# Attention, dense layers and routed experts in one kernel: ScalarE copies the gate columns, and the second batch's first head pair is prepared in the dense stage

## What is computed

```python
for t in range(S):                                  # attention, per batch and head
    cur = einsum('bhd,bhe->bhde', u[None] * kt, vt)
    y[:, :, t] = einsum('bhd,bhde->bhe', rt, state + cur)
    state = wt[:, :, :, None] * state + einsum('bhd,bhe->bhde', kt, vt)
x = y as [3072 tokens, 384]
h = ((x @ w1) * (x @ w2)) @ w3                      # dense, 384 -> 1024 -> 1024
x = h @ w_out                                       # -> 384
noisy = x @ w_gate + log1p(exp(x @ w_noise)) * noise
top2 of noisy per token, softmax of the two         # routing, 8 experts
out[token] += weight * (relu(x @ w1[e]) @ w2[e])    # for both chosen experts e
```

## Time and profile before

| | us |
|---|---|
| median of 3 runs | 1007.42 |
| lowest and highest | 1006.35, 1007.83 |
| the profiled execution, its own time | 1000.34 |
| its span in the profile | 998.6 |
| PE busy | 958.8 (96%) |
| DVE busy | 685.1 (69%) |
| ACT busy | 526.9 (53%) |
| first `up` of the first batch starts | 106.75 |
| first `up` of the second batch starts | 209.40 |

### The profile page before, as it was taken

How to read it: one execution, slowest core, us unless ns; L and a number is a source line. 1 busy time by engine, 2 the same in 40 slices (tenths; PEclk the granted TensorE clock), 3 DMA queues, 4 the chain that set the end, 5 groups by cost and what they waited for, 6 DMA issues and landing times.

```text
span 998.6 us, 18069 instructions
## 1 busy us (share of the span) xinstructions
PE 958.8 (96%) x6825; PEld 902.6 (90%) x6825; DVE 685.1 (69%) x1145; ACT 526.9 (53%) x986; POOL 223.9 (22%) x209
## 2 busy tenths in 40 slices
PE   4898999999999999999999999999999999999995
PEld 3555899999999999999999999999999999999995
DVE  7788786969797878263778585765857658576570
ACT  2543444445454635234545575665756657566560
POOL 0000100020202020203344323333332332323321
PEclk9998999999999999999999999999999999999998
DMA  8985524253435220306348797877968779787751
GB/s 257 281 252 159 169 80 133 87 180 94 130 103 172 73 70 29 101 1 220 115 169 264 198 298 210 245 255 210 304 206 246 253 213 299 207 246 254 211 158 16
DMA packets 87308, 179.02 MB, mean 179 GB/s; under 512 B 18915, under 2 KB 44261, under 8 KB 87221
## 3 DMA queue, kind: packets, MB, share of 16 engines
q1 hardware_dynamic: 73844, 157.18, 49.5%
q0 software_dynamic: 12976, 20.66, 9.9%
q10 hardware_dynamic: 400, 0.02, 0.0%
HBM read 152.22 MB, written 26.97 MB: 179 GB/s over the span
## 4 chain that ended last, share of the span: by engine, by line
PE 87%; DVE 7%; ACT 3%; issue 2%; POOL 0%; DVEq 0%; POOLq 0%; ACTq 0%
PE bank L1214 20%; PE pp L1230 20%; PE bank L785 11%; PE bank L802 7%; PE fx L785 6%; PE fx L802 4%; PE yu L1273 3%; PE pp L186 3%; DVE kdiv L258 2%; PE tr L1195 2%; PE yu L1255 1%; PE fx L1255 1%; PE fx L672 1%; PE yu L207 1%; PE yu L230 1%
## 5 line engine op out<-in xcount | busy, mean ns | idle before, releaser
L1123 POOL DMA_INDIRECT result<-x2s,who x55 | 92.9, 1689 | 284.5 <-ACT x2s L1347 265.2
L1334 DVE SCALAR_TENSOR_TENSOR abl<-bank,abh 128x512 fp32r<-128x512 f32 x96 | 66.2, 691 | 109.9 <-ACT abh L1329 109.9
L974 POOL DMA_INDIRECT slot_entry<-entry,slot_i x48 | 52.0, 1082 | 345.0 <-DVE token_f L963 332.9
L1214 PE MATMUL bank<-xh,set_up_h 128*128 128x256 f32 x384 | 109.2, 284 | 0.0
L1214 PE MATMUL bank<-xh,set_up_l 128*128 128x256 f32 x384 | 108.6, 283 | 0.0
L1214 PE MATMUL bank<-xl,set_up_h 128*128 128x256 f32 x384 | 108.6, 283 | 0.0
L1329 ACT ACTIVATE abh<-bank 128x512 fp32r<-128x512 f32 x96 | 57.5, 599 | 81.6 <-PE bank L1214 81.4
L312 ACT ACTIVATE att<-ident,diag 128x128 f32<-128x128 f32 x192 | 60.6, 392 | 69.5 <-DVE diag L297 69.5
L785 PE MATMUL bank<-xh,w12h 128*128 128x384 f32 x264 | 89.6, 339 | 1.7 <-DVE xl L481 1.5
L785 PE MATMUL bank<-xh,w12l 128*128 128x384 f32 x264 | 88.4, 335 | 0.0
L785 PE MATMUL bank<-xl,w12h 128*128 128x384 f32 x264 | 88.2, 334 | 0.0
(11 more groups left out here) (260 smaller groups left out, 2654.5 us busy)
## 6 DMA issues: line engine op xcount, KB each, us to landing
up_raw<-in_moe_w SPq DMA_DIRECT2D x93, 512.0 KB, 4.6
down_raw<-in_moe_w SPq DMA_DIRECT2D x124, 384.0 KB, 4.7
vs<-in_v_rows SPq DMA_DIRECT2D x16, 384.0 KB, 3.7
wt<-in_w SPq DMA_DIRECT2D x32, 144.0 KB, 2.9
kt<-in_k SPq DMA_DIRECT2D x32, 144.0 KB, 3.0
rt<-in_r SPq DMA_DIRECT2D x32, 144.0 KB, 3.4
kn<-in_k_rows SPq DMA_DIRECT2D x16, 288.0 KB, 2.9
rn<-in_r_rows SPq DMA_DIRECT2D x16, 288.0 KB, 3.5
```

Of the source, the lines that this page charges most:

```text
L974: nc.gpsimd.indirect_dma_start(slot_entry, bass.IndirectOffsetOnAxis(slot_i[:, s, n:n + 1], 0), entry[:, s, n, :], None).then_inc(scattere ...
L1123: nc.gpsimd.indirect_dma_start(out, bass.IndirectOffsetOnAxis(who[v % 4][:, s, 0:1], 0), yo[v % 2][:, s, 0:DM], None, bounds_check=N - 1, ...
L1214: last = nc.tensor.matmul(bank[m % 2][:, f * T2:(f + 1) * T2], wp[:, kk, c:c + P], xp[:, kk, :], start=(n == 0), stop=(n == 3 * KD - 1))
L1334: nc.vector.scalar_tensor_tensor(hl[:, 2 * m:2 * m + 2, :].rearrange("p a t -> p (a t)"), bank[m % 2][:, :], 0.0, hh[:, 2 * m:2 * m + 2, : ...
```

## The change

Two edits. First, the copy of the gate columns from `fx` into `wo` goes from DVE to ACT, in the same step `gates_turn`. Second, in the weight stage the steps of pair 4 (the second batch's first) are dropped from the slots and the last two slots are cut: 38 slots in place of 43, over which the same 29 quarters are dealt. The first dense batch gets the seven slots of `first_slots()` ahead of its 40, with pair 0 of the next batch in them. The batches after keep their list.

```diff
-TAIL = 3
+TAIL = 8
...
+        def own_slots(slots, pairs):
+            return [[step for step in slot if step[1] < pairs] for slot in slots]
...
-            order += threaded(build, [slot for q in range(HP) for slot in pair_slots(q, q == 0)] + [[]] * TAIL)
+            order += threaded(build, own_slots([slot for q in range(HP) for slot in pair_slots(q, q == 0)], HP)[:TAIL - 10])
...
+                    elif step == "gates_turn":            # first_act
+                        act.wait_ge(gates_full, 2)
+                        nc.scalar.copy(wo[:, :, DM:WA].rearrange("p (j t) e -> p t j e", t=2),
+                                       fx[:, 2 * P:4 * P].rearrange("p (t j e) -> p t j e", t=2, j=4)[:, :, :, 0:2 * E]
+                                       ).then_inc(wo_ready, 1)
...
-                    if step == "gates_turn":              # first_dve
-                        dve.wait_ge(gates_full, 2)
-                        nc.vector.tensor_copy(wo[:, :, DM:WA].rearrange("p (j t) e -> p t j e", t=2),
-                                              fx[:, 2 * P:4 * P].rearrange("p (t j e) -> p t j e", t=2, j=4)[:, :, :, 0:2 * E]
-                                              ).then_inc(wo_ready, 1)
...
-            both = threaded(group_steps(False), [slot for q in range(HP) for slot in pair_slots(q)])
+            every_slot = [slot for q in range(HP) for slot in pair_slots(q)]
+            both = [threaded(group_steps(False), first_slots() + every_slot if b == 0 else every_slot) for b in range(B - 1)]
...
-                    for step, q, n in both:               # on all five engines
+                    for step, q, n in both[b]:
```

More of the change, by code:

```diff
@@ L618, in first_dve @@
                     dve_attention(dve, 0, step, q, n)
-                    if step == "gates_turn":
-                        dve.wait_ge(gates_full, 2)
-                        nc.vector.tensor_copy(wo[:, :, DM:WA].rearrange("p (j t) e -> p t j e", t=2),
-                                              fx[:, 2 * P:4 * P].rearrange("p (t j e) -> p t j e", t=2, j=4)[:, :, :, 0:2 * E]
-                                              ).then_inc(wo_ready, 1)
-                    elif step == "w3_mm" and n == 2 and 1 <= q <= 2 * KD:
+                    if step == "w3_mm" and n == 2 and 1 <= q <= 2 * KD:
                         m, kk = divmod(q - 1, KD)
@@ L1502, in rest_act @@
                 for b in range(B - 1):
-                    for step, q, n in both:
+                    for step, q, n in both[b]:
                         if step in GROUP:
```

## The result

| | before | after |
|---|---|---|
| median of 4 runs, us | 1007.62 | 1013.55 |
| lowest and highest | 1006.35, 1008.55 | 1012.35, 1014.05 |
| the profiled execution, its own time | 1000.34 | 1012.35 |
| first `up` of the first batch | 106.75 | 101.80 |
| first `up` of the second batch | 209.41 | 215.19 |

The ratio is 1.0058, with a 95% interval of 1.004 to 1.0075: some 5.9 us slower, where I had forecast +1.4 and a range up to 1012.4. The two profiles give the same size up to the second batch's first `up`: 215.19 - 209.41 = +5.8. That they agree so well is in part luck: in the repeats that point lies 2.6 us later for before (e9) and 1.2 us later for the changed kernel (e5). The part behind it does the same work in both; its 6.2 us more in this one profile are no effect of the change (runs e2, e3 and e12).

A forecast was written before the change was run, and what follows sets the result against it. Before the first `up` PE and DVE take turns, neither full; from there PE is the bound. Terms -5.3 + 1.6 + 3.7 + 1.4 = +1.4 us on the median 1007.42 gave 1008.8, range 1003.4 to 1012.4.

The forecast's parts named there:

- the seam: Weight stage's end: first `up` at 101.4 instead of 106.75, -5.3 us (bounds -2.3 and -6.4).
- my two cases: Last pair of the weight stage: `out` 3.0 at 88.7 at full clock, or 92.7 if half clock comes back.
- score and keys: First dense batch: PE gets pair 0's score and keys, +1.6 us, fully on the bound engine.
- what the first dense batch costs: First dense batch: score and keys +1.6, PE's waits +3.7 and the clock +1.4 us.
- The clock: Behind the new 5 us wait before the first `up`: half clock expected, +1.4 us (0 to 3.2).
- my own walk: First dense batch, steps followed from the first `up`: PE waits 1.3 us before the second score, 1.4 before `state`, 0.5 once.
- PE's waits: First dense batch: PE waits for masks, `state` and other hand-overs, +3.7 us (bounds 1 and 7).
- (b): Weight stage's last pair: half clock comes back, `out` 3.0 at 92.7, total +4.4 us, 1011.8; chance 0.15.
- (d): Wait before the first `up`: longer clock drop, 3.2 us in place of 1.4, total +3.2, 1010.6; chance 0.10.
- (c): Weight stage: a late transfer of w3 or w1 eats the gate-column copy's 2.1 us, total +3.5, 1010.9; chance 0.08.
- (a): Weight stage at full clock, short drop at first `up`, dense batch stalls 1.5 us: -2.8, 1004.6; chance 0.27.
- The base: Whole kernel: the +1.4 us difference is put on the runs' median, 1007.42, not on the profiled execution's 1000.34.

The follow-up runs named there:

- e9: The kernel before run again with no edit: ratio 1.0006 to before.
- e5: The changed kernel run again with no edit: ratio 1.0062 to before.
- e2: The changed kernel plus 25 products that nobody reads in PE's wait before the first `up`: ratio 1.0028 to before.
- e3: The changed kernel with the `diag` steps first in the seven first slots of the first dense batch: ratio 1.0050 to before.
- e12: The changed kernel plus products that nobody reads, 25 before the first `up` and 18 before pair 0's second score: ratio 1.0019 to before.
- e8: The changed kernel with only pair 4's spreads moved, plus 25 products that nobody reads before the first `up`: ratio 0.9956 to before.
- e7: The changed kernel with an empty slot behind each of the seven preparation slots of the first dense batch: ratio 1.0070 to before.
- e4: The changed kernel with only pair 4's spreads moved, its `derive` and `diag` steps back in the weight stage: ratio 0.9961 to before.
- e1: The kernel before with only the gate columns' copy moved from DVE to ACT: ratio 0.9950 to before.
- e10: The kernel before with only the gate columns' copy moved to ACT, run again: ratio 0.9959 to before, median 997.31 us.
- e11: The changed kernel with only pair 4's spreads moved and 25 unread products before the first `up`, run again: ratio 0.9954 to before, median 996.73 us.

## Why the prediction was wrong

**Right: the bound and the seam.** `w3_mm` began at 17.90 (17.2 forecast), behind ACT's copy of 0.27 us (0.35). The first mask came at 25.01 (24.9). The half clock of 20 to 23 was gone. `out` 3.0 came at 90.35 (89.7 as a mean; 88.7 without half clock in the last pair, 92.7 with it): there was half clock, in the window below, which cost 1.7 us, so it lies between my two cases.

```profile
82.10:85.50 3.40, 3.40 (x10) 1.60 (x9) 2.24 (x2) 3.29 (x9) 0.00 (x0) 0.50 0.63 195
```

The read back was issued at 95.27 and the first `up` was at 101.80 (101.4), with 4.45 us of wait (5). The term was -5.3, measured -4.95 against the first profile of before; against its repeat (109.34) it would be -7.5, so the close agreement is partly luck. And edit 1 alone gained 4 to 5 us by the runs where I gave it 2.1, which fits the first profile of before and not the repeat.

**Right: score and keys.** +1.6 forecast; e8, where nothing else is left, shows 1.3.

**Wrong, the step that failed: what the first dense batch costs, 6.7 forecast and 10.7 measured.** Two of its three terms were too small, each by some 2 us.

**The clock, "+1.4" (0 to 3.2), measured 3.4.** 1.7 us were lost behind the seam, as forecast; but the 3.2 us wait inside the batch brought a second stretch at 1.2 GHz, 1.7 us more. I had priced the clock for the wait that I saw as idle time and not for the wait that my own walk made. This term lies outside its own bounds. In e5, with the longer stretch behind the seam, it was 4.3. e12 gets 3.0 of the 3.4 back by filling the two waits.

**PE's waits, "+3.7" (1 to 7), measured 6.1, of which before had 0.5: +5.6.** The parts that I named add up to 4.2 (1.3 before the second score, 1.4 before `state`, 0.5 once, 1.0 for the rest); 3.7 is right only with before's 0.5 taken off, which the text doesn't say. In the first pair the walk was near: 2.7 forecast, 3.2 measured, all of it before the second score and none before `state`. e2 shows that part at full clock: there the reduction ended 14.9 us behind the first `up` (14.6 in the walk), but the first mask 19.1 us behind it (17.6). In the walk the mask followed two spreads, while DVE's list has the multiply and low part of `up` 7 ahead of it, and these wait for ACT's copy of `up` 6, which the order puts behind the same two spreads. I had followed ACT's list for the keys' copy and not for this one; no run puts that copy ahead of the spreads. The larger miss is behind the first pair: 1.5 us forecast, 2.8 measured (0.6 at a `down`, 1.3 at an `up`, 0.8 at the last pair's `state`, 0.2 elsewhere). I judged that part by DVE's share. The load was forecast well, 89.5 us and 89.4 measured; but that is a share of 0.79 of the longer batch, less than the second batch's 0.82, where PE is idle for 0.9 us. So the share doesn't tell the waits. e7 suggests that the waits are one quantity: with room at the start 6.1 us of them moved to the end. No run shows why it is the same number.

Sum of the batch: 1.6 + 5.6 + 3.4 = 10.6, measured 10.7. With the seam's -4.95 this is the +5.8 of the profiles.

The rules of the Trainium skill that the prediction weighed (TensorE: Matmul & The Clock Gate, HAM oscillation; Loop structure matters more than you think) say that idle stretches bring the array's clock down and that a long wait ahead of the products makes them run cold. The profiles here agree: every wait of 3.2 us or more at or behind the seam in the changed kernel was followed by half clock, and the batch had none where PE had products to do in these waits (e8, e12). Shorter waits were followed by it too: 2.45 and 2.07 us in e7.

**The rivals.** (b) named as its sign more than 2 us at 0.5 between score and `out` of the last pair, and these came (82.1 to 85.5); but `out` 3.0 was then 1.65 us late and not 4, and the first `up` at 101.8 and not 104.4. So its total, 1011.8, is near the measured one by luck: the loss was made in the dense batch. (d) comes nearest: a longer loss to the clock, here from two drops and not one; in e4 to e7 the drop at the seam was itself as long as (d) has it, some 7 us. (c) did not happen. (a) was wrong; yet e4 and e8 show where its gain lay: DVE's 8.23 idle us ahead of the read back, in which the removed preparation fits.

**The base.** I put the difference on the median, and that base held (1007.42, then 1007.62), since the result's runs of before are the same three and one more. The profile of before was no picture of them: it was 2.6 us better ahead of the first `up` than its repeat, and the part behind differed by 3 to 6 us between sets of runs. Spans of profiles could not be compared; up to an instruction that both have they could, to within the 1 to 3 us by which the half clock moves it.

## What to carry to other kernels

Work that is moved out of a stage bound by a helper engine into one bound by PE is not free because the helper shows 20% of idle time there (here it cost 5.6 us of waits): write down each hand-over, in every engine's list, and compare the helper's passes between two hand-overs with PE's. If the helper idles while data travel, as DVE did here before the read back, leave its work there and move only what stands in the way of the next transfer's consumer. And give every wait of some 3 us that the plan makes the price of the half clock behind it, 1.7 us or more here.

## What was not expected of the hardware

Edit 1 was worth 4 to 5 us though it moves a copy of 0.28 us and shortens a wait by 3.2: removing the early wait also removes the half clock behind it (20 to 23 in the first profile, 19 to 26 in the repeat). That accounts for 2.3 to 3.8 us: the second pair's scans, the next link of the chain, begin at 32.51 and 34.00 in the two profiles of before and at 30.16 and 30.17 in e1 and e10. What makes the rest is not shown; e9 has another stretch of half clock from 46.6. Stretches of half clock lasted from 3.5 to 7 us in profiles of the same kernel, and the same kernel's first `up` came 2.6 us apart in two executions of before, 1.6 in two of edit 1 alone.

From the second batch's first `up` to the end the program took 789.2 to 789.7 us in two sets of runs and in the first profile of before, and 792.6 to 795.7 in the third set and the first changed profile, whatever the kernel. In the changed kernel's first profile PE waits there 2.7 us for DVE at L1219, which the profile of before does not show. It is not the change's: e8 and e11 are the same program, and e8 has these waits where e11 has none. What sets it was not tried.
